# Two first pieces in whole float32, and weights split over four stages instead of three

## The chip, the cores and the metric

The kernel runs on one core of a Trainium2 chip. The metric is the device time of one execution in microseconds (us). A core has five engines that run side by side, each through its own instructions in the order in which they are written: TensorE (PE in the profile; its weight loads are PEld), VectorE (DVE), ScalarE (ACT), GpSimd (POOL) and SyncE (SP, which issues every transfer here). They wait for each other through semaphores.

## The reference

```python
scores = q @ k.transpose(0, 1, 3, 2) / 8             # 4 batches, 8 heads, 576 tokens, 64 a head
kth = np.partition(scores, -32, axis=-1)[..., -32:-31]
attn = softmax(np.where(scores >= kth, scores, -1e9))  # the 32 largest of each row
x = (attn @ v) as 2304 tokens of 512
x = (sigmoid(x @ w_gate) * (x @ w_val)) @ w_out       # 512 -> 1536 -> 512
out = np.maximum(x @ w_in, 0) ** 2 @ w_out2           # 512 -> 2048 -> 512
```

All of it is float32.

## The kernel before

The 2304 tokens are worked in six **pieces** of 192, 384, 448, 512, 512 and 256 tokens. The attention of a piece runs ahead of its two feed-forward layers, and the attention of later pieces runs beside the layers of earlier ones.

**Attention** goes by 144 *tiles* of 128 query rows, for one head, or for two heads with 64 rows each. A tile's scores are made on PE (`score`, L402), copied out by ACT (L529), and seven passes on DVE find its 32 largest (`select`, L661 and L663). ACT and POOL turn that into masked and normalised probabilities (L534 to L551, L728, L733). PE transposes them (`turn`, L418) and multiplies them by v (`times_v`, L438). ACT copies the result to x (`copy_x`). The program is written in 150 *slots*. In slot s, DVE selects tile s, PE makes the scores of tile s + 3, and POOL masks tile s - 2 and normalises tile s - 3.

**The layers** go by 68 *blocks* of weights (512 x 128) for each piece: 24 `gate` and `val`, 12 `y`, 16 `h`, 16 `out`. PE takes a block in two halves. `MLP_AT` names the slot in which a piece's layers begin (16, 41, 69, 101, 133 and 149), and `shares` deals its halves out evenly over the slots up to the next piece's. Those of the last piece come after everything (`REST`). Three PSUM banks take the sums in turn, and DVE, ACT and POOL empty them (`evac`).

The first piece multiplies whole float32 values (L483). The others split each operand into two float32r parts, high and low, and sum three products (L497 to L499). Weights get to that form once: ACT writes the high part of a block (L575), POOL the low part (L723), and SP stores both to `w_split` in HBM (`store_parts`, L337); later pieces load them from there (L332). A third of the blocks is split before the first piece's layers, a third during that piece, right after PE has used the block whole, and a third during the second piece, five blocks ahead of use.

Blocks pass through a **ring** of eight places. SP walks the blocks in order. At block k it first loads block k + 7 into the place that block k - 1 leaves, and then stores the parts of block k if it is one of the split ones:

```python
load_weights(k - 1 + RING)
...
if c == 0 and k in SPLIT_OF:
    store_parts(k)
```

`load_weights` waits in `wait_place` until PE is done with the block that held the place (`blk_done`) and, where that block was split, until its store has landed (`w_stored`, L301). `store_parts` waits for POOL's low part.

Of the kernel before, what the change touches and what calls it, by code (L numbers as in the profile page):

```python
# [25 lines left out]
CHUNK_BLOCKS = (3, 6, 7, 8, 8, 4)  # L26
NC = len(CHUNK_BLOCKS)
WIDTH = [B64 * n for n in CHUNK_BLOCKS]
# [66 lines left out]
JOBS = [(None, n, True, True) for n in range(0, NB, 3)]  # L95
NPRE = len(JOBS)
JOBS += [(c, n, c < 2 and c == n % 3 - 1, c == 0 or c == 1 and n % 3 == 2) for c in range(NC) for n in range(NB)]

SPLITS = sorted((k for k in range(len(JOBS)) if JOBS[k][2]), key=lambda k: k - (AHEAD + 0.5 if JOBS[k][0] == 1 else 0))
# [11 lines left out]
MLP_AT = [CHUNK_END[c] + (6 if c else 5) for c in range(NC)]  # L111
# [60 lines left out]
for _c in range(1, NC):  # L172
# [10 lines left out]
def attention_mlps(nc, qk, v, w, w_split, out):  # L183
    with ExitStack() as ctx:
# [15 lines left out]
        probs_h = sb("probs_h", [P, SEQ + B64])  # L200
# [11 lines left out]
        g_hi = sb("g_hi", [P, NJ2, NMAX], F32R)  # L212
        g_lo = sb("g_lo", [P, NJ2, NMAX], F32R)
# [11 lines left out]
        T0, LAST, PV, ACC0 = 2, 4, P, 5  # L225

# [14 lines left out]
        def probs_of(t):  # L241
            u, part = TILES[t]
            return probs_h[:, 0:SEQ] if part == 2 else probs[:, RANK[u] % 2, part, :]
# [62 lines left out]
        def _(sp):  # L306
# [33 lines left out]
            def mlp_dma(blocks):  # L340
                for c, n in blocks:
                    kind, m, i, parts = BLOCKS[n]
                    k = NPRE + c * NB + n

                    load_weights(k - 1 + RING)
                    if k + AHEAD in SPLIT_OF and JOBS[k + AHEAD][0] == 1:
# [34 lines left out]
        def _(pe):  # L381
# [24 lines left out]
            def turn(u):  # L406
                pe.wait_ge(norm_done, END[u] + 1)
                wait(pe, pt_copied, u)

                wait(pe, s_copied, max([t + 1 for t in range(NT) if TILES[t][1] == 1  # L410
                                        and FIRST_OF[TILES[t][0]] - SCORE <= END[u] + TURN], default=0))

                wait(pe, x_done, u)
                half = UNITS[u][4]
                both = probs_h if half else probs[:, RANK[u] % 2, :, :].rearrange("p h c -> p (h c)")
# [26 lines left out]
            def mlp_half(c, half):  # L442
                n = half // 2
                kind, t, i, parts = BLOCKS[n]
                if i == 0 and half % 2 == 0:
                    a = c * NA + ACC_OF[n] - NACC
                    before, (kind_a, ta) = a // NA, ACCS[a % NA]
                    if a < 0:
                        pass
                    elif kind_a == "gate":  # L450
                        pe.wait_ge(tanh_done, before * NJ1 + ta + 1)
                    elif kind_a == "val":
                        pe.wait_ge(gv_done, before * NJ1 + ta + 1)
                    elif kind_a == "y":
                        if before == 0:
                            pe.wait_ge(y_hi_done, ta + 1)
                        else:
                            pe.wait_ge(y_lo_done, (before - 1) * NM + ta + 1)
                    elif kind_a == "h":
                        pe.wait_ge(relu_done, before * NJ2 + ta + 1)  # L460
                    else:
                        pe.wait_ge(out_copied, before * NM + ta + 1)
                job = NPRE + c * NB + n
                if half % 2 == 0:
                    if c == 1 and job in SPLIT_OF:
                        pe.wait_ge(w_lo_done, SPLIT_OF[job] + 1)
                    else:
                        pe.wait_ge(ring_loaded[job % RING], 16 * (job // RING + 1))
                dst = acc(c, n)
                for kt in range(half % 2 * KT // 2, (half % 2 + 1) * KT // 2):  # L470
                    k = i * KT + kt
                    first, final = k == 0, k == parts * KT - 1
                    if c == 0:
                        if n == 0:
                            pe.wait_ge(x_done, X_UNIT[0][k] + 1)
                        elif kind == "y" and t == 0:
                            pe.wait_ge(gv_done, k + 1)
                        elif kind == "h" and t == 0:
                            pe.wait_ge(y_hi_done, k + 1)
                        elif kind == "out" and t == 0:  # L480
                            pe.wait_ge(sq_done, k + 1)
                        data = g0 if kind in ("y", "out") else y0 if kind == "h" else x0
                        mm = nc.tensor.matmul(dst, whole(job)[:, kt * P:kt * P + P], data[:, k, 0:WIDTH[c]],  # L483
                                              start=first, stop=final)
                        continue
                    if n == 0:
                        pe.wait_ge(x_lo_done, (c - 1) * NM + k + 1)
                    elif kind == "y" and t == 0:
                        pe.wait_ge(gv_lo_done, (c - 1) * NJ1 + k + 1)
                    elif kind == "h" and t == 0:  # L490
                        pe.wait_ge(y_lo_done, (c - 1) * NM + k + 1)
                    elif kind == "out" and t == 0:
                        pe.wait_ge(sq_lo_done, (c - 1) * NJ2 + k + 1)
# [30 lines left out]
        def _(act):  # L524
# [39 lines left out]
            def copy_x(u):  # L564
                c, g, p, i, half, col = UNITS[u]
                act.wait_ge(pv_done, u + 1)
                if c > 1:

                    act.wait_ge(x_lo_done, (c - 2) * NM + p + 1)
                x, n = (x0 if c == 0 else xf), (B64 if half else P)  # L570
# [11 lines left out]
            def evac(c, n):  # L582
# [3 lines left out]
                if k + AHEAD in SPLIT_OF and JOBS[k + AHEAD][0] == 1:  # L586
                    split_weights(k + AHEAD)
                if c == 0 and k in SPLIT_OF:
                    split_weights(k)
                if i == parts - 1 and kind != "val":  # L590
# [8 lines left out]
                    elif kind == "y":  # L599
                        y = y0 if c == 0 else xy_hi  # L600
# [8 lines left out]
                if c > 0 and 2 <= n <= 2 * NJ1 and n % 2 == 0:  # L609
# [3 lines left out]
                if c > 0 and H0 < n <= OUT0:  # L613
# [36 lines left out]
        def _(dve):  # L650
# [27 lines left out]
            def evac(c, n):  # L678
                kind, t, i, parts = BLOCKS[n]
                n_w = WIDTH[c]  # L680
                if kind == "val":
                    dve.wait_ge(blk_done, c * NB + n + 1)
                    dve.wait_ge(tanh_done, c * NJ1 + t + 1)
                    if c > 0 and t >= 2:
                        dve.wait_ge(gv_lo_done, (c - 1) * NJ1 + t - 1)
                    gv = g0[:, t, 0:n_w] if c == 0 else full_buf[:, t % 2, 0:n_w]
# [3 lines left out]
                if c > 0 and kind == "y" and i == parts - 1:  # L690
# [4 lines left out]
                if c > 0 and H0 + 2 <= n < OUT0 + 2:  # L695
                    j = n - H0 - 2
                    dve.wait_ge(sq_hi_done, (c - 1) * NJ2 + j + 1)
# [20 lines left out]
        def _(pool):  # L718
            def split_weights(k):
                pool.wait_ge(w_hi_done, SPLIT_OF[k] + 1)  # L720
                if JOBS[k][0] == 0:
# [15 lines left out]
            def split_x(c, p):  # L737
                pool.wait_ge(x_hi_done, (c - 1) * NM + p + 1)
# [4 lines left out]
            def evac(c, n):  # L743
                n_w = WIDTH[c]
                k = NPRE + c * NB + n
                if k + AHEAD in SPLIT_OF and JOBS[k + AHEAD][0] == 1:
                    split_weights(k + AHEAD)
                if c == 0 and k in SPLIT_OF:
                    split_weights(k)
                if c > 0 and 2 <= n <= 2 * NJ1 and n % 2 == 0:  # L750
                    j = n // 2 - 1
                    pool.wait_ge(gv_hi_done, (c - 1) * NJ1 + j + 1)
# [3 lines left out]
                if H0 <= n < OUT0:  # L756
                    j = n - H0
                    pool.wait_ge(relu_done, c * NJ2 + j + 1)
                    if c > 0 and j >= 2:
                        pool.wait_ge(sq_lo_done, (c - 1) * NJ2 + j - 1)  # L760
                    elif c > 0:
                        pool.wait_ge(gv_lo_done, (c - 1) * NJ1 + NJ1 - 1 + j)
                    sq = g0[:, j, 0:n_w] if c == 0 else full_buf[:, j % 2, 0:n_w]
# [4 lines left out]
            nc.gpsimd.memset(probs_h[:, :], 0.0).then_inc(const_step, 1)  # L768
# [69 lines left out]
```

## Time and profile before

| | |
|---|---|
| runs of the kernel | 1252.79, 1248.31, 1250.70 us; median 1250.7 |
| the profiled execution | 1252.19 us, of which 1250.4 us from the first instruction to the last |
| busy in that span | PE 1169.2, DVE 848.4, ACT 740.7, POOL 626.3 us |
| mean granted TensorE clock | 0.978 of full speed |
| moved by DMA | 270 MB |

Busy time overlaps between engines; a busy PE also counts the drain of one matmul beside the start of the next. A stage of the program is best read by its own window: how long it lasted, which engine was busy in all of it, and what the others waited for.

### The profile page before, as it was taken

The page shows a single profiled execution, that of the slowest core. Times are in us where ns is not written, and L with a number is a line of the kernel's source. Part 1 is how long each engine was busy: PE and PEld are TensorE (multiplying, and loading weights), DVE is VectorE, ACT ScalarE, POOL GpSimd, SP SyncE. Part 2 cuts the span into 40 slices and gives each one's busy share as a digit, 9 for nine tenths or more (in the row PEclk, how much of TensorE's full clock was granted, in tenths as well). Part 3 has the DMA queues.
Part 4 walks back from the last instruction along what each step waited for, and adds up shares of the span by engine and source line. Part 5 has one row for each costly group of instructions (what it writes and reads, how often), then busy time and mean ns, then how long its engine had stood idle before and what let it go on. Part 6 is the DMA issues. An engine that isn't in the chain of part 4 may idle for free.

```text
span 1250.4 us, 21797 instructions
## 1 busy us (share of the span) xinstructions
PE 1169.2 (94%) x7520; PEld 991.9 (79%) x7520; DVE 848.4 (68%) x1756; ACT 740.7 (59%) x1758; POOL 626.3 (50%) x539
## 2 busy tenths in 40 slices
PE   3469989869999999999999999999999999999999
PEld 2248877769999898888888777777778788888999
DVE  7988988737779977788997667688864445610121
ACT  5777778557768756666776666467654443531221
POOL 4875668646648845553664445356543333530220
PEclk9769999989999999999999999999999999999999
DMA  7874667686665785655456555454555545556997
GB/s 262 313 266 143 230 209 225 204 298 225 224 228 199 246 309 192 198 199 170 160 191 230 200 168 191 168 185 153 175 193 194 178 160 181 176 189 212 365 369 263
DMA packets 89245, 270.13 MB, mean 216 GB/s; under 512 B 9904, under 2 KB 15024, under 8 KB 89136
## 3 DMA queue, kind: packets, MB, share of 16 engines
q1 hardware_dynamic: 89136, 268.74, 62.7%
q8 instruction: 61, 1.00, 0.4%
q14 instruction: 48, 0.39, 0.1%
HBM read 228.33 MB, written 40.37 MB: 215 GB/s over the span
## 4 chain that ended last, share of the span: by engine, by line
PE 80%; ACT 6%; POOL 4%; DMA 4%; DVE 4%; issue 2%; SPq 1%; ACTq 0%; DVEq 0%; POOLq 0%
PE ps L497 21%; PE ps L499 19%; PE ps L498 19%; PE ps L438 6%; PE ps L402 5%; PE ps L418 5%; PE ps L483 3%; DMA w_split<-ring 2%; POOL below L728 2%; DVE work L663 2%; DVE top L661 1%; POOL ring L723 1%; ACT scores L529 1%; DMA ring<-w_in 1%; ACT probs L548 1%
## 5 line engine op out<-in xcount | busy, mean ns | idle before, releaser
L728 POOL TENSOR_TENSOR below<-scores,below 128x576 f32<-128x576 f32 x144 | 205.2, 1425 | 297.9 <-ACT below L541 285.5
L661 DVE MAX8 top<-work 128x8 f32<-128x576 f32 x432 | 312.9, 752 | 5.0
L497 PE MATMUL ps<-xy_hi,ring 128*128 128x512 f32 (+3 forms) x800 | 292.1, 365 | 0.3 <-ACT act_buf L597 0.3
L499 PE MATMUL ps<-xy_hi,ring 128*128 128x512 f32 (+3 forms) x800 | 283.2, 354 | 0.0
L498 PE MATMUL ps<-xy_lo,ring 128*128 128x512 f32 (+3 forms) x800 | 283.2, 354 | 0.0
L663 DVE MATCH_REPLACE8 work<-top,work 128x576 f32<-128x576 f32 x288 | 213.8, 742 | 0.0
L497 PE MATMUL ps<-g_hi,ring 128*128 128x512 f32 (+3 forms) x560 | 203.0, 363 | 0.0
L499 PE MATMUL ps<-g_hi,ring 128*128 128x512 f32 (+3 forms) x560 | 197.8, 353 | 0.0
L498 PE MATMUL ps<-g_lo,ring 128*128 128x512 f32 (+3 forms) x560 | 197.6, 353 | 0.0
L497 PEld LDWEIGHTS ps<-xy_hi,ring 128*128 128x128 f32 x800 | 151.4, 189 | 24.8 <-issue 9.7
L687 DVE SCALAR_TENSOR_TENSOR full_buf<-act_buf,ps 128x512 f32<-128x512 f32 (+3 forms) x60 | 35.5, 591 | 193.1 <-PE ps L499 176.7
L499 PEld LDWEIGHTS ps<-xy_hi,ring 128*128 128x128 f32 x800 | 151.4, 189 | 15.9
L498 PEld LDWEIGHTS ps<-xy_lo,ring 128*128 128x128 f32 x800 | 151.7, 190 | 14.1
L733 POOL TENSOR_TENSOR probs<-probs,rinv 128x576 f32<-128x576 f32 x128 | 153.2, 1197 | 16.3 <-DVE rinv L676 15.9
L548 ACT ACTIVATE probs<-below,nbias 128x576 f32<-128x576 f32 x128 | 100.1, 782 | 66.6 <-POOL below L728 65.0
L753 POOL TENSOR_TENSOR g_lo<-full_buf,g_hi 128x512 fp32r<-128x512 f32 (+3 forms) x60 | 65.8, 1096 | 126.3 <-ACT g_hi L612 126.3
L402 PE MATMUL ps<-heads_in 64*128 64x288 f32 (+1 forms) x640 | 103.3, 469 | 17.6 <-ACT scores L529 8.0
L497 PEld LDWEIGHTS ps<-g_hi,ring 128*128 128x128 f32 x560 | 105.6, 189 | 16.9 <-issue 7.0
L418 PE MATMUL ps<-ident,probs 128*128 128x128 f32 x576 | 79.9, 288 | 40.5 <-POOL probs L733 20.9
L499 PEld LDWEIGHTS ps<-g_hi,ring 128*128 128x128 f32 x560 | 105.6, 189 | 11.0
L723 POOL TENSOR_TENSOR ring<-ring 128x512 fp32r<-128x512 f32 x68 | 87.2, 1289 | 53.9 <-ACT ring L575 43.2
L534 ACT ACTIVATE below<-scores,top 128x576 f32<-128x576 f32 x144 | 111.7, 776 | 3.8 <-DVE top L661 3.5
(56 smaller groups left out, 1749.9 us busy)
## 6 DMA issues: line engine op xcount, KB each, us to landing
ring<-w_split SPq DMA_DIRECT2D x318, 512.0 KB, 3.7
w_split<-ring SPq DMA_DIRECT2D x68, 512.0 KB, 4.2
ring<-w_in SPq DMA_DIRECT2D x113, 256.0 KB, 3.4
vt<-v_in SPq DMA_DIRECT2D x16, 480.0 KB, 5.3
heads_in<-qk_in SPq DMA_DIRECT2D x16, 336.0 KB, 4.8
vt<-v_in SPq DMA_DIRECT2D x16, 320.0 KB, 4.1
heads_in<-qk_in SPq DMA_DIRECT2D x16, 240.0 KB, 3.8
heads_in<-qk_in SPq DMA_DIRECT2D x8, 368.0 KB, 5.6
```

The source lines that it names most:

```text
L402: mm = nc.tensor.matmul(ps[out_rows, score_bank(t) + half, 0:HALF], heads_in[rows, r, P * i:P * i + n], heads_in[rows, r, q:q + HALF], sta ...
L418: mm = nc.tensor.transpose(dst, both[:, P * k:P * k + P], ident[:, :])
L497: nc.tensor.matmul(dst, w_hi, hi[:, k, 0:WIDTH[c]], start=first, stop=False)
L498: nc.tensor.matmul(dst, w_hi, lo[:, k, 0:WIDTH[c]], start=False, stop=False)
L499: mm = nc.tensor.matmul(dst, w_lo, hi[:, k, 0:WIDTH[c]], start=False, stop=final)
L534: nc.scalar.activation(below[:, t % 2, :], scores[:, t % PLACES, :], ACT.Sign, bias=top[:, t % 4, TOPK - 1:TOPK], scale=-1.0).then_inc(sig ...
L548: nc.scalar.activation(probs_of(t), below[:, t % 2, :], ACT.Exp, bias=nbias[:, t % 4:t % 4 + 1], scale=SCALE, accum_out=rsum[:, t % 4:t % ...
L661: nc.vector.max(out=best, in_=sc if step == 0 else wk).then_inc(sel_step[t % 2], 1)
L663: nc.vector.match_replace(out=wk, in_to_replace=best, in_values=sc if step == 1 else wk, imm_value=-3.0e38).then_inc(sel_step[t % 2], 1)
L723: nc.gpsimd.tensor_tensor(out=place(k)[:, 1, :], in0=whole(k), in1=place(k)[:, 0, :].bitcast(F32), op=ALU.subtract).then_inc(w_lo_done, 1)
L728: nc.gpsimd.tensor_tensor(out=below[:, t % 2, :], in0=scores[:, t % PLACES, :], in1=below[:, t % 2, :], op=ALU.subtract).then_inc(mask_don ...
L733: nc.gpsimd.tensor_tensor(out=probs_of(t), in0=probs_of(t), in1=rinv[:, t % 4:t % 4 + 1].to_broadcast([P, SEQ]), op=ALU.mult).then_inc(nor ...
```

## The change

The pieces become 128, 192, 448, 512, 512 and 512 tokens, and the layers begin in slots 12, 24, 53, 85, 117 and 149. The first two pieces (`NW = 2`) multiply whole float32 values. The second of them keeps its x in a buffer of its own, `x1`, laid over `g_lo`, which is first written in the third piece. The weights are split in fourths: before the layers (17 blocks), during the first, the second and the third piece (17 each). `probs_h` gets two buffers. The work of one tile and of one block is as it was.

```diff
-CHUNK_BLOCKS = (3, 6, 7, 8, 8, 4)
+CHUNK_BLOCKS = (2, 3, 7, 8, 8, 8)
+NW = 2
...
-JOBS = [(None, n, True, True) for n in range(0, NB, 3)]
+CLASSES = NW + 2
+JOBS = [(None, n, True, True) for n in range(0, NB, CLASSES)]
...
-JOBS += [(c, n, c < 2 and c == n % 3 - 1, c == 0 or c == 1 and n % 3 == 2) for c in range(NC) for n in range(NB)]
+JOBS += [(c, n, c + 1 == n % CLASSES, c < NW or c == NW and n % CLASSES == CLASSES - 1)
+         for c in range(NC) for n in range(NB)]
...
-MLP_AT = [CHUNK_END[c] + (6 if c else 5) for c in range(NC)]
+MLP_AT = [CHUNK_END[c] + (5 if c < NW else 6) for c in range(NC)]
...
-        each = 2 * (WIDTH[c] / 0.6 + 6) if c == 0 else 6 * max(WIDTH[c] / 2.33 + 10, 110)
+        each = 2 * (WIDTH[c] / 0.6 + 6) if c < NW else 6 * max(WIDTH[c] / 2.33 + 10, 110)
...
-        probs_h = sb("probs_h", [P, SEQ + B64])
+        probs_h = sb("probs_h", [P, 2, SEQ + B64])
...
+        with nc.sbuf_tensor("x1", [P, NM, NMAX], F32) as x1:
+            pass
...
+        def x_of(c):
+            return (x0, x1)[c] if c < NW else xf
...
-                    if c == 0 and k in SPLIT_OF:
+                    if c < NW and k in SPLIT_OF:
                         store_parts(k)
...
-                    if c == 0:
+                    if c < NW:
                         if n == 0:
-                            pe.wait_ge(x_done, X_UNIT[0][k] + 1)
+                            pe.wait_ge(x_done, X_UNIT[c][k] + 1)
```

Elsewhere `c == 0` becomes `c < NW`, `c == 1` becomes `c == NW`, and counts of semaphores that start with the first split piece start at `NW`.

On PE, the start of the first piece's layers. Before, from the transposes of tile 9 on; the L483 rows are the layers, counted as the program writes them (the trace has two records for each float32 multiplication), with x as the moving operand:

```order
L418 MATMUL ps<-ident,probs 128x128 x9
L438 MATMUL ps<-pt,vt 64x128 x10
L418 MATMUL ps<-ident,probs_h 128x128 x5
L402 MATMUL ps<-heads_in 128x288 x4
L438 MATMUL ps<-pt,vt 64x64 x10
L483 MATMUL ps<-x,ring 128x192 x14
L418 MATMUL ps<-ident,probs 128x128 x9
L483 MATMUL ps<-x,ring 128x192 x2
L402 MATMUL ps<-heads_in 128x288 x4
L438 MATMUL ps<-pt,vt 64x128 x10
L483 MATMUL ps<-x,ring 128x192 x20
```

The same place after the change, where L428, L448, L412 and L493 are the lines that were L418, L438, L402 and L483:

```order
L428 MATMUL ps<-ident,probs 128x128 x9
L412 MATMUL ps<-heads_in 128x288 x4
L448 MATMUL ps<-pt,vt 64x128 x10
L493 MATMUL ps<-x,ring 128x128 x26
L428 MATMUL ps<-ident,probs 128x128 x9
L493 MATMUL ps<-x,ring 128x128 x6
L412 MATMUL ps<-heads_in 64x288 x4
L448 MATMUL ps<-pt,vt 64x128 x10
L493 MATMUL ps<-x,ring 128x128 x14
L428 MATMUL ps<-ident,probs_h 128x128 x5
L493 MATMUL ps<-x,ring 128x128 x8
```

The layers now begin after four units of probabilities instead of eight, on 128 columns instead of 192, and each stretch between two pieces of attention work holds more of them.

On SP, the middle of the first piece's layers. Before, `ring<-w_in` being the load of a whole block, `w_split<-ring` the store of a split one:

```order
L328 DMA ring<-w_in 128x512 x3
L337 DMA w_split<-ring 128x1024
L328 DMA ring<-w_in 128x512 x3
L337 DMA w_split<-ring 128x1024
L328 DMA ring<-w_in 128x512 x3
L337 DMA w_split<-ring 128x1024
L328 DMA ring<-w_in 128x512
L312 DMA heads_in<-qk_in 128x736 x2
L328 DMA ring<-w_in 128x512 x2
L337 DMA w_split<-ring 128x1024
```

After, with L338 and L347 for L328 and L337:

```order
L338 DMA ring<-w_in 128x512 x4
L347 DMA w_split<-ring 128x1024
L338 DMA ring<-w_in 128x512 x4
L347 DMA w_split<-ring 128x1024
L338 DMA ring<-w_in 128x512 x2
L322 DMA heads_in<-qk_in 128x544 x2
L338 DMA ring<-w_in 128x512 x2
L347 DMA w_split<-ring 128x1024
```

Between two stores there are now four loads instead of three, and the same order runs through the second piece as well.

## Rows read from the trace of the kernel before

**Rows 1.** The page: busy us of each engine, share of the span, instructions.

```profile
PE 1169.2 (94%) x7520; PEld 991.9 (79%) x7520; DVE 848.4 (68%) x1756; ACT 740.7 (59%) x1758; POOL 626.3 (50%) x539
```

**Rows 2.** Windows by stage: length, busy by engine, clock, DMA share, GB/s.

```profile
0.00:95.50 95.50, 46.45 (x313) 30.26 (x313) 82.23 (x176) 66.64 (x154) 63.90 (x57) 0.79 0.78 275
95.50:257.70 162.20, 141.92 (x1007) 123.24 (x1006) 132.61 (x290) 116.64 (x293) 103.71 (x94) 0.97 0.63 209
257.70:463.60 205.90, 199.19 (x1387) 181.03 (x1385) 164.66 (x342) 143.44 (x345) 132.39 (x112) 0.99 0.70 243
463.60:690.80 227.20, 225.73 (x1418) 194.57 (x1417) 186.70 (x387) 151.41 (x356) 117.24 (x97) 1.00 0.58 194
690.80:920.00 229.20, 228.07 (x1393) 177.50 (x1393) 171.54 (x351) 146.24 (x338) 113.30 (x89) 1.00 0.53 179
920.00:1149.60 229.60, 229.60 (x1203) 187.41 (x1198) 93.97 (x180) 93.17 (x209) 77.13 (x64) 1.00 0.55 182
1149.60:1250.40 100.80, 98.23 (x817) 97.92 (x816) 16.68 (x32) 23.20 (x65) 18.64 (x28) 1.00 0.89 328
```

**Rows 3.** Waits of SP's queue from 143.8 to 249.2: total us, times, longest.

```profile
SPq L301 <- DMA w_split<-ring: 67.7, 14, 6.2
```

**Rows 4.** Timeline of SP's queue in the first piece: start, length, issue.

```profile
113.16 0.33 SPq L337 DMA_DIRECT2D w_split<-ring  x1
115.81 1.28 SPq L328 DMA_DIRECT2D ring<-w_in  x3
...
143.77 1.28 SPq L328 DMA_DIRECT2D ring<-w_in  x3
...
164.00 1.28 SPq L328 DMA_DIRECT2D ring<-w_in  x3
165.32 0.43 SPq L337 DMA_DIRECT2D w_split<-ring  x1
170.28 0.33 SPq L328 DMA_DIRECT2D ring<-w_in  x1
...
249.22 0.32 SPq L332 DMA_DIRECT2D ring<-w_split  x1
```

**Rows 5.** The chain that ended last, 95 to 280: two of its links.

```profile
157.63 2.73 DMA ring<-w_in
...
214.64 6.61 DMA w_split<-ring
```

**Rows 6.** DVE timeline: first pass on tiles 12 and 16; below, that pass from 102.9 to 181.

```profile
68.65 0.74 DVE L661 MAX8 top<-scores 128x8 f32<-128x576 f32 x1
...
93.30 0.74 DVE L661 MAX8 top<-scores 128x8 f32<-128x576 f32 x1
...
L661 DVE MAX8 top<-scores x15: 740/743/744, 103.0 to 180.9; 128x8 f32<-128x576 f32 x15
```

**Rows 7.** PE timeline: the first layer matmuls, and 36 in a row without a wait.

```profile
95.47 4.23 PE L483 MATMUL ps<-x,ring 128*128 128x192 f32 x24
...
118.09 6.12 PE L483 MATMUL ps<-x,ring 128*128 128x192 f32 x36
124.05 1.15 PE L418 MATMUL ps<-ident,probs 128*128 128x128 f32 x9
```

**Rows 8.** PE timeline: first and last of 20 neighbours of 512 columns.

```profile
1130.14 0.39 PE L498 MATMUL ps<-g_lo,ring 128*128 128x512 f32 x1
...
1134.46 0.39 PE L499 MATMUL ps<-g_hi,ring 128*128 128x512 f32 x1
```

**Rows 9.** Windows: within the last piece, and around the second piece's first matmul.

```profile
1180.00:1220.00 40.00, 40.00 (x335) 39.94 (x334) 9.08 (x17) 11.30 (x32) 9.41 (x15) 1.00 0.98 368
...
250.00:275.00 25.00, 16.43 (x97) 14.66 (x97) 8.60 (x20) 10.99 (x26) 9.84 (x8) 0.86 0.86 305
```

**Rows 10.** Timeline of the end: PE's last matmul, and the last output's transfer.

```profile
1247.55 0.28 PE L499 MATMUL ps<-g_hi,ring 128*128 128x256 f32 x1
...
1248.28 0.34 SPq L352 DMA_DIRECT2D out<-act_buf  x1
```

More of the change, by code:

```diff
@@ L94 @@
 AHEAD = 5
-JOBS = [(None, n, True, True) for n in range(0, NB, 3)]
+CLASSES = NW + 2
+JOBS = [(None, n, True, True) for n in range(0, NB, CLASSES)]
 NPRE = len(JOBS)
-JOBS += [(c, n, c < 2 and c == n % 3 - 1, c == 0 or c == 1 and n % 3 == 2) for c in range(NC) for n in range(NB)]
-SPLITS = sorted((k for k in range(len(JOBS)) if JOBS[k][2]), key=lambda k: k - (AHEAD + 0.5 if JOBS[k][0] == 1 else 0))
+JOBS += [(c, n, c + 1 == n % CLASSES, c < NW or c == NW and n % CLASSES == CLASSES - 1)
+         for c in range(NC) for n in range(NB)]
+SPLITS = sorted((k for k in range(len(JOBS)) if JOBS[k][2]), key=lambda k: k - (AHEAD + 0.5 if JOBS[k][0] == NW else 0))
 SPLIT_OF = {k: r for r, k in enumerate(SPLITS)}
@@ L171 @@
     HEADS_AT.setdefault(max(FIRST_TILE[_g - 1] - 3, 0), []).append(_g)
-for _c in range(1, NC):
+for _c in range(NW, NC):
     for _p in range(PAIRS):
@@ L242, in probs_of @@
             u, part = TILES[t]
-            return probs_h[:, 0:SEQ] if part == 2 else probs[:, RANK[u] % 2, part, :]
+            return probs_h[:, RANK[u] % 2, 0:SEQ] if part == 2 else probs[:, RANK[u] % 2, part, :]
         def place(k):
@@ L414, in turn @@
                 half = UNITS[u][4]
-                both = probs_h if half else probs[:, RANK[u] % 2, :, :].rearrange("p h c -> p (h c)")
+                both = probs_h[:, RANK[u] % 2, :] if half else probs[:, RANK[u] % 2, :, :].rearrange("p h c -> p (h c)")
                 for k in range(KFULL + 1 if half else NBLK):
@@ L454, in mlp_half @@
                     elif kind_a == "y":
-                        if before == 0:
-                            pe.wait_ge(y_hi_done, ta + 1)
+                        if before < NW:
+                            pe.wait_ge(y_hi_done, before * NM + ta + 1)
                         else:
-                            pe.wait_ge(y_lo_done, (before - 1) * NM + ta + 1)
+                            pe.wait_ge(y_lo_done, (before - NW) * NM + ta + 1)
                     elif kind_a == "h":
@@ L464, in mlp_half @@
                 if half % 2 == 0:
-                    if c == 1 and job in SPLIT_OF:
+                    if c == NW and job in SPLIT_OF:
                         pe.wait_ge(w_lo_done, SPLIT_OF[job] + 1)
@@ L566, in copy_x @@
                 act.wait_ge(pv_done, u + 1)
-                if c > 1:
-                    act.wait_ge(x_lo_done, (c - 2) * NM + p + 1)
-                x, n = (x0 if c == 0 else xf), (B64 if half else P)
+                if c > NW:
+                    act.wait_ge(x_lo_done, (c - NW - 1) * NM + p + 1)
+                x, n = x_of(c), (B64 if half else P)
                 nc.scalar.activation(x[:, p, col:col + n], ps[:, LAST, PV:PV + n], ACT.Copy).then_inc(x_done, 1)
@@ L585, in evac @@
                 k = NPRE + c * NB + n
-                if k + AHEAD in SPLIT_OF and JOBS[k + AHEAD][0] == 1:
+                if k + AHEAD in SPLIT_OF and JOBS[k + AHEAD][0] == NW:
                     split_weights(k + AHEAD)
-                if c == 0 and k in SPLIT_OF:
+                if c < NW and k in SPLIT_OF:
                     split_weights(k)
@@ L599, in evac @@
                     elif kind == "y":
-                        y = y0 if c == 0 else xy_hi
+                        y = y0 if c < NW else xy_hi
                         nc.scalar.activation(y[:, t, 0:n_w], acc(c, n), ACT.Copy, scale=0.5).then_inc(y_hi_done, 1)
@@ L608, in evac @@
                         nc.scalar.activation(act_buf[:, t % 2, 0:n_w], acc(c, n), ACT.Copy).then_inc(out_copied, 1)
-                if c > 0 and 2 <= n <= 2 * NJ1 and n % 2 == 0:
+                if c >= NW and 2 <= n <= 2 * NJ1 and n % 2 == 0:
                     j = n // 2 - 1
@@ L612, in evac @@
                     nc.scalar.activation(g_hi[:, j, 0:n_w], full_buf[:, j % 2, 0:n_w], ACT.Copy).then_inc(gv_hi_done, 1)
-                if c > 0 and H0 < n <= OUT0:
+                if c >= NW and H0 < n <= OUT0:
                     j = n - H0 - 1
@@ L683, in evac @@
                     dve.wait_ge(tanh_done, c * NJ1 + t + 1)
-                    if c > 0 and t >= 2:
-                        dve.wait_ge(gv_lo_done, (c - 1) * NJ1 + t - 1)
-                    gv = g0[:, t, 0:n_w] if c == 0 else full_buf[:, t % 2, 0:n_w]
+                    if c >= NW and t >= 2:
+                        dve.wait_ge(gv_lo_done, (c - NW) * NJ1 + t - 1)
+                    gv = g0[:, t, 0:n_w] if c < NW else full_buf[:, t % 2, 0:n_w]
                     nc.vector.scalar_tensor_tensor(out=gv, in0=act_buf[:, t % 2, 0:n_w],
@@ L689, in evac @@
                                                    op1=ALU.mult).then_inc(gv_done, 1)
-                if c > 0 and kind == "y" and i == parts - 1:
+                if c >= NW and kind == "y" and i == parts - 1:
                     dve.wait_ge(y_hi_done, c * NM + t + 1)
@@ L720, in split_weights @@
                 pool.wait_ge(w_hi_done, SPLIT_OF[k] + 1)
-                if JOBS[k][0] == 0:
+                if JOBS[k][0] is not None and JOBS[k][0] < NW:
                     pool.wait_ge(blk_done, k - NPRE + 1)
@@ L758, in evac @@
                     pool.wait_ge(relu_done, c * NJ2 + j + 1)
[L759 to L763, printed above, removed]
+                    if c >= NW and j >= 2:
+                        pool.wait_ge(sq_lo_done, (c - NW) * NJ2 + j - 1)
+                    elif c >= NW:
+                        pool.wait_ge(gv_lo_done, (c - NW) * NJ1 + NJ1 - 1 + j)
+                    sq = g0[:, j, 0:n_w] if c < NW else full_buf[:, j % 2, 0:n_w]
                     nc.gpsimd.tensor_tensor(out=sq, in0=act_buf[:, j % 2, 0:n_w],
@@ L767, in _ @@
             nc.gpsimd.memset(ident[:, :], 0.0)
-            nc.gpsimd.memset(probs_h[:, :], 0.0).then_inc(const_step, 1)
+            nc.gpsimd.memset(probs_h[:, :, :], 0.0).then_inc(const_step, 1)
             pool.wait_ge(const_step, 1)
```

32 lines of the change are left out of this document (16 added, 16 removed).

## The prediction

> **What bounds the kernel now.** The page comes first: PE is busy 94% of the span [rows 1]. That is an average over unlike stages, so the next view is the windows by stage [rows 2]. From 463.6 us on PE is busy in 225.7 of 227.2 us, then 228.1 of 229.2, 229.6 of 229.6, 98.2 of 100.8: there PE's amount of work is the time. Before that it is not. Up to 95.5 us there is only attention, with PE busy 46.5 us. In the first piece's layers PE is busy 141.9 of 162.2 us, in the second piece's 199.2 of 205.9.
>
> Who sets the pace of the first piece? SP's waits say it [rows 3]: from 143.8 to 249.2 us SP stood 67.7 us, 14 times, until a store to `w_split` had landed. The timeline shows the cycle [rows 4]: three loads at 164.00, a store at 165.32, and the next load only at 170.28, because its place in the ring is the one being stored; SP issues in order, so every load behind it stands too. From 143.77 to 249.22 that is 15 cycles, 7.03 us each for three blocks, 2.34 us a block, attention's own loads included. PE needs less. 36 neighbouring records take 5.96 us [rows 7], 0.1655 each, so a block of eight is 1.32 us. Attention costs PE 1.83 us a slot: a pass of 512 columns takes 4.32 / 19 = 0.2274 us [rows 8], a piece has 816, and the two pieces from 690.8 to 1149.6 us with 48 slots give (458.8 - 371.1) / 48. At the stage's mean of 162.2 / 25 = 6.5 us a slot, 16 slots passed in those 105 us, so PE had 45 x 1.32 + 16 x 1.83 = 89 us to do. The chain agrees: it runs through a store at 214.64 and a load at 157.63 [rows 5].
>
> **The change, stage by stage.** All sums are against the span of 1250.4 us.
>
> *Start of the layers.* It moves from slot 16 to slot 12. DVE starts tile 12 at 68.65 and tile 16 at 93.30 [rows 6], and the first layer matmul follows the latter by 2.2 us [rows 7]. I put the new start at 70 us: 25.5 gained. Six blocks fewer are split before it, which may bring 67; more and shorter head loads may cost up to 78.
>
> *First piece, 128 tokens.* Proportional to columns a record takes 0.110 us, 544 of them 60 us; if it got no shorter than at 192 columns, 90. With 12 slots of attention PE's need is 82 us (112 at most). But the piece still walks 68 blocks, with 17 stores among them, and between two stores stand four loads. The shortest cycle is 7.03 plus one issue of 0.43, that is 7.46. The longest grows with the bytes, from 1.31 to 1.57 MB: 8.4. I take the 0.26 MB at the 368 GB/s that the last piece reaches [rows 9], 0.71 us: 7.75 us for four blocks, against PE's 4 x 82 / 68 = 4.8. SP therefore sets this stage. The last block's load stands behind the fifteenth store: 4.5 us to the first store, 14 cycles, and 11 us for that store, three issues, the landing and the last block. That is 4.5 + 108.5 + 11 = 124 us (120 to 134). Behind the late blocks on PE stand the scores of the next tiles, so DVE idles here: 12 slots in 124 us.
>
> The Trainium skill ("DMA: Bandwidth & Descriptors", Anatomy of one DMA) fits a DMA, on the GpSimd path, as about 2.0 us plus bytes over 436 GB/s, which is an estimate of 3.2 us for this store. The store at 113.16 landed within 2.65 us, near that, but with three loads just ahead of it in the queue it takes 5.0. By the skill's price the stage would last some 90 us and the sum would be 1232.
>
> *Second piece, 192 tokens in float32.* PE: 544 x 0.1655 = 90, plus 29 slots x 1.83 = 53: 143 us. The stores' chain, 17 cycles of 7.75, is 132 us and hidden. The pace is DVE's: from 103.0 to 180.9 us, beside a piece of the same width, 14 slots took 77.9 us, 5.56 each [rows 6]; 29 slots are 161.5 us. Bounds: 29 slots of seven passes of 0.743 us are 151, and the first piece's 6.5 us a slot would make 188.
>
> *Third piece, 448 tokens, 32 slots.* The same piece took 227.2 us before [rows 2]. It now also has the 17 splits ahead of use that the second piece had, and that piece began badly: from 250 to 275 us PE was busy 16.4 us [rows 9], because the ring was empty behind the stores. Here the ring is full before it, as the second piece leaves the chain slack. I add 7: 234 (228 to 244).
>
> *Fourth and fifth piece, 512 each.* PE-bound before and after; they now carry 64 slots of attention instead of 48: 371.1 + 64 x 1.83 = 488 us. DVE's 64 x 5.56 us are hidden.
>
> *Last piece, 512 instead of 256.* No attention is left: 816 x 0.2274 = 185.5 us. The tail after PE's last matmul, 2.9 us [rows 10], grows to about 3.5 with twice the output: 189, against 100.8. DMA, at 0.98 share before [rows 9], gets slack, but PE was never short of a block there, so that pays nothing.
>
> `x1`, the second `probs_h` and the shifted counts add no instruction. POOL clears twice as much of `probs_h` at the start, behind the first transfer of heads; uncovered that would shift the start by its own length, within the start's bounds.
>
> Sum: 70 + 124 + 161.5 + 234 + 488 + 189 = 1266.5 us, 16 more than the span before. Or in two halves: the start gains 25.5, the float32 pieces take 285.5 where one took 162.2, and what is left takes 911 instead of 992.7: -25.5 + 123.3 - 81.7 = +16. The profiled execution lay 1.8 us over its span and 1.5 over the median of the runs, so the median should be about 1267.
>
> **The rivals.**
>
> *The stores land as if alone (faster).* If each lands within 3 us, as at 113.16, a cycle is 5 x 0.43 + 3.0 = 5.2 us, the chain needs 4.5 + 14 x 5.2 + 9 = 86 us, near PE's 82, and the stage lasts about 90. It decides from a cycle of 4.8 us down that PE alone sets the stage. Everything else unchanged: 1232. For it: the trace has such stores. Against it: they came when SP had waited for something else first; in saturation the 14 waits averaged 4.8 us. 0.18. The Trainium skill's fit, above, amounts to this case.
>
> *The second piece falls behind.* At the first piece's mean of 6.5 us a slot it takes 188 us: 1293. For it: waits in order on five engines add up. Against it: the later slots of that stage were held by SP's chain, which here has 30 us of slack. 0.12.
>
> *The clock falls.* With PE idle for a third of the first piece, it may be granted the lower of its levels, 1.2 GHz, in much of it. From 250 to 275 us, with PE busy 16.4 us, the mean was 0.86; before the layers it was 0.79 [rows 2]. At half clock throughout, PE needs 2 x 82 = 164 us, 40 more than SP: 1306. Short drops are covered by SP's waits. 0.06.
>
> *The forecast*, stores in saturation: 0.64, in a range of its own from 1249 to 1284 (the bounds above, not all at one end at once).
>
> **The numbers.** A change under 0.3%, 3.8 us, cannot be told from none here, as the three runs lie 0.36% apart. Faster, under 1247: the first rival and a sliver of the forecast, 0.20. Within: the forecast's lower edge, and a first piece halfway to the rival, 0.12. Slower: the rest, 0.68. The range from 1238 to 1290 leaves out most of the first rival, the third, and the upper end of the second.
>
> **What would show it.** The first layer matmul at 67 to 78 us. SP's waits for `w_split` stores filling most of the first piece, cycles near 7.75 us with four loads, PE waiting for `ring<-w_in` there and DVE busy about half. The second piece's layers begin near 194 us and last about 160, with DVE near full. PE busy all through from the third piece on, the last piece 189 us. The prediction is wrong if cycles in the first piece come near 5 us, or if the second piece is paced by anything but DVE.

## The result, and the profile after

The change makes the kernel slower: 1291.5 us median of four runs (1289.06 to 1293.95) against 1250.3, a ratio of 1.0334 (95% interval 1.0313 to 1.0355). The direction was forecast, the size was not: 41 us instead of 16, and 1.5 us beyond the range. The profiled execution took 1291.94 us, with a span of 1290.1.

The page, with the rows that answer to [rows 1] and the slices of PE's busy time:

```profile
PE 1185.0 (92%) x7248; PEld 975.1 (76%) x7248; DVE 838.9 (65%) x1736; ACT 734.1 (57%) x1726; POOL 618.2 (48%) x523
...
PE   2587667999989999999999999999999999999999
```

The windows by stage, in the columns of [rows 2]: before the layers, the first, second and third piece, the fourth and fifth together, the last piece with the tail.

```profile
0.00:77.60 77.60, 35.79 (x188) 23.33 (x188) 63.24 (x133) 48.32 (x108) 47.00 (x43) 0.81 0.75 267
77.60:208.90 131.30, 97.67 (x819) 87.51 (x817) 64.87 (x146) 65.66 (x170) 58.16 (x58) 0.93 0.66 216
208.90:375.40 166.50, 149.45 (x1132) 128.53 (x1130) 148.23 (x329) 123.78 (x315) 104.46 (x94) 0.98 0.66 219
375.40:613.10 237.70, 229.83 (x1419) 197.54 (x1417) 188.61 (x387) 162.63 (x379) 142.37 (x117) 0.99 0.62 218
613.10:1101.90 488.80, 487.18 (x2886) 385.13 (x2885) 345.56 (x711) 296.85 (x689) 234.09 (x186) 1.00 0.52 171
1101.90:1290.10 188.20, 185.11 (x817) 153.01 (x815) 28.43 (x32) 36.90 (x65) 32.06 (x28) 1.00 0.54 178
```

Beside the forecast's terms of 70, 124, 161.5, 234, 488 and 189 us stand 77.6, 131.3, 166.5, 237.7, 488.8 and 188.2. The two PE-bound terms fit within 1 us. The first four are all too small, by 7.6, 7.3, 5.0 and 3.7 us, together 23.6.

In the first piece SP's waits, as in [rows 3], are for the stores again: 76.7 us in 15 waits.

```profile
SPq L311 <- DMA w_split<-ring: 76.7, 15, 6.7
SPq L347 <- POOL ring L733: 7.2, 2, 5.5
```

PE's own waits in that stage show what this does, which before had been 7.7 us between 143.8 and 249.2:

```profile
PE ps L493 <- DMA ring<-w_in: 30.5, 21, 3.4
```

SP's timeline, to be read as [rows 4], has the cycle of four loads and a store. The first store of the piece is at 85.15, 7.5 us after the first matmul; the fifteenth, at 196.09, comes 14 cycles later, (196.09 - 85.15) / 14 = 7.92 us each:

```profile
85.15 0.33 SPq L347 DMA_DIRECT2D w_split<-ring  x1
...
161.52 1.75 SPq L338 DMA_DIRECT2D ring<-w_in  x4
163.31 0.43 SPq L347 DMA_DIRECT2D w_split<-ring  x1
169.13 1.75 SPq L338 DMA_DIRECT2D ring<-w_in  x4
...
196.09 0.44 SPq L347 DMA_DIRECT2D w_split<-ring  x1
```

PE's timeline at the start shows the third group's scores waiting for their heads. At the start of the second piece it shows a wait for a block, and behind it a longer one for ACT; at the start of the third a wait for ACT alone:

```profile
14.90 2.29 PE L412 MATMUL ps<-heads_in 64*128 64x288 f32 x8 [5.67 <-DMA heads_in<-qk_in]
...
77.61 2.65 PE L493 MATMUL ps<-x,ring 128*128 128x128 f32 x17
...
208.90 1.47 PE L493 MATMUL ps<-x,ring 128*128 128x192 f32 x8
212.54 1.70 PE L493 MATMUL ps<-x,ring 128*128 128x192 f32 x9 [2.17 <-DMA ring<-w_in]
...
222.61 1.33 PE L412 MATMUL ps<-heads_in 64*128 64x288 f32 x4 [4.91 <-ACT pt L572]
...
381.74 0.76 PE L412 MATMUL ps<-heads_in 64*128 64x288 f32 x4 [4.23 <-ACT pt L572]
```

Both waits for ACT lead back to SP's queue. In the second piece ACT could not empty one of its first sums into `act_buf`, because an output of the first piece was still to be read from there, and SP issued that transfer only after it had stood for a store. In the third piece ACT stood for a block that it was to split. SP's timeline, then ACT's:

```profile
212.13 0.43 SPq L347 DMA_DIRECT2D w_split<-ring  x1
217.37 0.80 SPq L338 DMA_DIRECT2D ring<-w_in  x2
218.22 0.43 SPq L362 DMA_DIRECT2D out<-act_buf  x1
```

```profile
220.99 0.33 ACT L607 ACTIVATE act_buf<-ps 128x192 f32<-128x192 f32 x1 [5.17 <-DMA out<-act_buf]
...
377.70 1.15 ACT L585 ACTIVATE ring<-ring 128x512 fp32r<-128x512 f32 x2 [3.32 <-DMA ring<-w_in]
```

### The profile page after: what moved, and what is told of

Read it like the earlier page. It is cut to its first block, busy times and chain, and to the rows that moved or that the text cites. A ratio compares the mean times of both kernels' runs of the same rounds, so it can differ in the third digit from the quotient of the medians.

```text
span 1290.1 us, 21141 instructions
## 1 busy us (share of the span) xinstructions
PE 1185.0 (92%) x7248; PEld 975.1 (76%) x7248; DVE 838.9 (65%) x1736; ACT 734.1 (57%) x1726; POOL 618.2 (48%) x523
## 4 chain that ended last, share of the span: by engine, by line
PE 77%; ACT 8%; DMA 7%; POOL 4%; issue 3%; DVE 1%; SPq 1%; ACTq 0%; POOLq 0%; DVEq 0%
PE ps L507 19%; PE ps L509 18%; PE ps L508 18%; PE ps L448 7%; PE ps L412 6%; PE ps L493 6%; PE ps L428 4%; DMA ring<-w_in 4%; DMA w_split<-ring 3%; POOL below L738 2%; ACT below L544 1%; ACT scores L539 1%; ACT probs L558 1%; ACT ring L585 1%; ACT below L551 1%
## 5 line engine op out<-in xcount | busy, mean ns | idle before, releaser
L507 PE MATMUL ps<-xy_hi,ring 128*128 128x512 f32 (+1 forms) x640 | 253.0, 395 | 0.0
L509 PE MATMUL ps<-xy_hi,ring 128*128 128x512 f32 (+1 forms) x640 | 246.1, 385 | 0.0
L508 PE MATMUL ps<-xy_lo,ring 128*128 128x512 f32 (+1 forms) x640 | 246.1, 385 | 0.0
L507 PE MATMUL ps<-g_hi,ring 128*128 128x512 f32 (+1 forms) x448 | 176.6, 394 | 0.0
L509 PE MATMUL ps<-g_hi,ring 128*128 128x512 f32 (+1 forms) x448 | 172.2, 384 | 0.0
L508 PE MATMUL ps<-g_lo,ring 128*128 128x512 f32 (+1 forms) x448 | 172.0, 384 | 0.0
L507 PEld LDWEIGHTS ps<-xy_hi,ring 128*128 128x128 f32 x640 | 120.3, 188 | 28.4 <-issue 8.3
L509 PEld LDWEIGHTS ps<-xy_hi,ring 128*128 128x128 f32 x640 | 120.3, 188 | 22.1
L412 PE MATMUL ps<-heads_in 64*128 64x288 f32 (+1 forms) x640 | 104.0, 467 | 30.5 <-ACT pt L572 17.1
L697 DVE SCALAR_TENSOR_TENSOR full_buf<-act_buf,ps 128x512 f32<-128x512 f32 (+1 forms) x48 | 32.0, 668 | 149.9 <-PE ps L509 149.9
L448 PEld LDWEIGHTS ps<-pt,vt 128*64 128x64 f32 x1600 | 86.2, 145 | 35.5 <-issue 24.1
L763 POOL TENSOR_TENSOR g_lo<-full_buf,g_hi 128x512 fp32r<-128x512 f32 (+1 forms) x48 | 60.3, 1257 | 109.0 <-ACT g_hi L622 109.0
L671 DVE MAX8 top<-scores 128x8 f32<-128x576 f32 x144 | 107.0, 743 | 5.9 <-ACT scores L539 5.9
L774 POOL TENSOR_TENSOR full_buf<-act_buf 128x512 f32<-128x512 f32 (+1 forms) x64 | 66.2, 1039 | 92.1 <-ACT act_buf L615 81.5
```

What stands on the lines that cost most here:

```text
L412: mm = nc.tensor.matmul(ps[out_rows, score_bank(t) + half, 0:HALF], heads_in[rows, r, P * i:P * i + n], heads_in[rows, r, q:q + HALF], sta ...
L448: mm = nc.tensor.matmul(ps[DH * h:DH * h + DH, LAST, PV:PV + n], vt[:, g % 2, v_at:v_at + DH], pt[:, u % 2, p_at:p_at + n], start=(k == 0) ...
L507: nc.tensor.matmul(dst, w_hi, hi[:, k, 0:WIDTH[c]], start=first, stop=False)
L508: nc.tensor.matmul(dst, w_hi, lo[:, k, 0:WIDTH[c]], start=False, stop=False)
L509: mm = nc.tensor.matmul(dst, w_lo, hi[:, k, 0:WIDTH[c]], start=False, stop=final)
L671: nc.vector.max(out=best, in_=sc if step == 0 else wk).then_inc(sel_step[t % 2], 1)
```

## The experiments

The theory: SP's wait for each store, in order ahead of the next loads, paces the first piece and makes the second begin late. Rivals: the engines' waits on each other pace it; the transfers' own time does; the width of the piece does. Stage lengths below run from a piece's first layer matmul to the next one's. They come from one profiled execution of each kernel; five of the kernels (no stores, thirds, both short ones and the 128 columns) were run only once. Where an edit leaves a stage alone, it repeats well: with the change the third piece took 237.7, and in three kernels edited elsewhere 237.7 to 238.4 us. The start of the layers scatters more, from 76.2 to 78.8 us in eight kernels with the same work before it.

**No stores in the first piece.**

```diff
-JOBS += [(c, n, c + 1 == n % CLASSES,
+JOBS += [(c, n, 0 < c and c + 1 == n % CLASSES,
...
+KEPT = [n - (n % CLASSES == 1) for n in range(NB)]
...
-                             w_split[n, :, :])
+                             w_split[KEPT[n], :, :])
```

> The changed kernel without any split or store during the first piece; later pieces load a neighbour's stored block in place of those 17, so their values are not the reference's while every transfer keeps its size. If SP's wait for the stores paces the first piece, that piece falls from 131 us to PE's need, 82 to 95 us, and SP waits for PE there instead; the second piece then begins on a full ring and loses its slow first slots, 166 to about 156 us. Span about 1240 to 1250. If the engines' waits on each other in order pace it, the piece stays over 115 us and the span over 1270.

The span fell to 1237.5 us, just under the expected. Windows of the first three pieces:

```profile
76.20:164.90 88.70, 85.56 (x819) 79.42 (x817) 64.73 (x146) 55.55 (x153) 36.64 (x41) 0.99 0.74 240
164.90:322.00 157.10, 146.51 (x1132) 126.10 (x1130) 148.22 (x329) 123.80 (x315) 104.81 (x94) 1.00 0.67 223
322.00:560.50 238.50, 231.06 (x1420) 198.28 (x1417) 188.61 (x387) 162.65 (x379) 142.34 (x117) 0.98 0.61 215
```

and SP's longest wait in the first of them:

```profile
SPq L339 <- PE ps L494: 51.5, 57, 3.2
```

SP now waits for PE, and the first piece takes 88.7 us with PE busy 85.6 of them. So the 17 stores (with their splits) cost the first piece 131.3 - 88.7 = 42.6 us and the second 166.5 - 157.1 = 9.4 more, though the second piece's own stores are unchanged. The third piece, behind those, keeps its 238.

**Thirds again, widths unchanged.**

```diff
-CLASSES = NW + 2
+CLASSES = NW + 1
...
-    SPLIT_AT.setdefault(2 + _k // 2, []).append(_k)
+    SPLIT_AT.setdefault(2 + 10 * _k // NPRE, []).append(_k)
```

> The changed kernel with the weights split in thirds again (before the layers, in the first and in the second piece, up to three a slot before the layers), widths unchanged. The first two pieces then have 23 stores each with three loads between them. If the number of stores paces the first piece, whatever its width, it rises from 131 us to 150 to 160, near the 162 that a piece of 192 tokens took before; the second piece is then near its own limit by the stores, 165 to 175. If the width paces it, it stays near 131 us. The third piece should lose its 4 us over the old one.

Span 1309.7 us. The first two windows:

```profile
79.10:231.10 152.00, 108.25 (x819) 96.42 (x818) 65.16 (x146) 68.18 (x176) 65.49 (x64) 0.85 0.69 224
231.10:401.10 170.00, 150.18 (x1130) 128.61 (x1129) 148.68 (x329) 127.24 (x322) 111.32 (x100) 0.98 0.67 230
```

The first two came as expected, the third piece, at 231.6 us, lost 6.1. A piece of 128 tokens with 23 stores takes 152 us, nearer to the 162 of 192 tokens with 23 stores [rows 2] than to its own 131 with 17: the number of stores weighs more than the width, 21 us against 10. Splitting in fourths was by itself a gain, of 20 us.

**The reload four blocks later, behind the next store.** In this edit and the next of its kind, `split_late(k)` is true for the blocks that are split after use.

```diff
+                    if not split_late(k - 1):
-                    load_weights(k - 1 + RING)
+                        load_weights(k - 1 + RING)
...
                         store_parts(k)
+                    if split_late(k - CLASSES):
+                        load_weights(k - CLASSES + RING)
```

> The changed kernel with the same work and the same stores; only SP's order differs: the load into the place of a block that is being stored is issued after the next store, four blocks later, so that the three loads behind it no longer stand. If the in-order wait is the cause, the first piece takes 90 to 105 us, the second about 156, and the span is 1245 to 1262. If the transfers themselves are the limit (their bytes and landing times), the first piece stays near 125 to 131 us and the span within 10 us of 1290.

1294.4 us, 1.035 times the kernel before (1.030 to 1.039): no gain, the first piece 132.2 us and the second 175.4. That looks like the rival, transfers as the limit. But SP's waits in the piece had changed their object:

```profile
SPq L347 <- POOL ring L739: 76.1, 17, 8.3
SPq L338 <- PE ps L499: 11.7, 21, 1.3
```

SP no longer waits for a store, it waits for POOL's low part of the next block to be stored. That block's load now lay behind a store in the queue, only four blocks ahead, so PE got it late (PE waited for loads 30.7 us in that piece), POOL after PE, and the store after POOL: another loop through the same place, of the same length.

**The reload three blocks later, ahead of the next store.**

```diff
+                    if not split_late(k - 1):
-                    load_weights(k - 1 + RING)
+                        load_weights(k - 1 + RING)
+                    if split_late(k - 3):
+                        load_weights(k - 3 + RING)
...
                         store_parts(k)
```

> The changed kernel, same work; the load into the place of a stored block is issued three blocks later, ahead of the next store and not behind it as in the run before. If the stand-still of SP in order was the cost, and the last try only swapped it for a load that lay behind a store and reached PE late, a cycle of four blocks shrinks from 7.9 to about 6 us, the first piece to 98 to 112 us and the span to 1250 to 1270. If the transfers' own time paces the cycle, the piece stays over 125 us.

The profiled span was 1250.5 us. Its pieces:

```profile
77.10:184.00 106.90, 91.55 (x821) 83.70 (x818) 65.61 (x147) 64.84 (x170) 57.45 (x57) 0.95 0.81 271
184.00:342.00 158.00, 146.71 (x1132) 126.02 (x1130) 148.21 (x329) 124.63 (x318) 105.17 (x94) 1.00 0.69 230
342.00:573.40 231.40, 226.49 (x1420) 195.09 (x1417) 187.66 (x387) 161.96 (x378) 142.47 (x117) 1.00 0.63 222
```

With every store and every byte kept, 24.4 us go from the first piece, 8.5 from the second and 6.3 from the third. The cycle of four blocks is 6.3 us. The transfers were not the limit; DMA now moves 271 GB/s there instead of 216. Not all of the cost is gone: the piece is 18 us longer than without stores, and SP still waited 32.0 us for stores in it and 20.5 us for POOL. The profiled execution was the fastest of five (1252.3 to 1263.1); their median, 1258.8, is 1.0077 times the kernel before (1.0042 to 1.0112).

**The first piece's splits moved to the third piece.**

```diff
-JOBS += [(c, n, c + 1 == n % CLASSES, c < NW or c == NW and n % CLASSES == CLASSES - 1)
+JOBS += [(c, n, c == 1 and n % 4 == 2 or c == NW and n % 2 == 1, c < NW or c == NW and n % 2 == 1)
```

> The changed kernel with the first piece's 17 splits moved into the third piece (34 there, five blocks ahead of use); nothing is left out. First piece 87 to 95 us, second about 157, third 242 to 252 as each 17 splits cost it about 6 us; the span 1240 to 1252, so the change without stores in its first piece is even with the kernel before or up to 0.8% faster. If splits ahead of use cost as much as those in the first piece, the third piece grows by 40 us and nothing is won.

1245.4 us, 0.9962 of the kernel before (0.9945 to 0.9979). First piece 90.3, second 157.1, third 241.0: with 17 more splits ahead of use that piece is 2.5 us longer than in the run without stores, not 6. Pieces and widths of the change, with the stores out of the first piece, are thus a small gain over the kernel before, and 46 us better than as written.

**Heads ahead of half of the first weights.**

```diff
-            for k in range(RING):
+            for k in range(RING // 2):
                 load_weights(k)
...
+                if s == 1:
+                    for k in range(RING // 2, RING):
+                        load_weights(k)
```

> The changed kernel with four of the first eight weight loads issued one slot later, behind the heads of the third and fourth group, for which PE waits 5.7 us now. If that wait is what made the slots before the layers 5.6 to 7 us long instead of 5.1, the first layer matmul comes at 70 to 73 us instead of 77.6 and the span falls by 4 to 7 us. If ACT and POOL are simply full in these slots, the start stays at 76 to 78 us and the span too.

1289.4 us, 1.0318 (1.0272 to 1.0364) of the kernel before; the span was 1285.2 instead of 1290.1, but the medians are only 2.1 us apart, within the scatter of either kernel. The layers began at 73.9 us instead of 77.6, just above the expected: by this run the wait for heads explains 3.7 of the 7.6 us by which the start missed.

**Moved splits and heads together.** The edits of the last two runs in one kernel.

> The changed kernel with the first piece's splits in the third piece and with four of the first weight loads behind the heads, nothing left out. The two gains lie in different stages: start 73 to 74 us, first piece 89 to 91, the rest as with the splits moved alone; span 1236 to 1241, 0.6 to 1.1% under the kernel before. If the earlier start is eaten by the first piece, the span stays at 1242.

1242.2 us, 0.9938 (0.9919 to 0.9957). The start is at 74.8 where the moved splits alone had 77.1, so here the heads are worth 2.3 us; the first piece takes 90.3 us. The two gains add up, nearly.

**Selection of the second piece's tiles cut short.**

```diff
-                sc, wk, tp = scores[:, t % PLACES, :], work[:, t % 2, :], top[:, t % 4, :]
+                cols = B64 if step > 3 and MLP_AT[1] <= t < MLP_AT[2] else SEQ
+                sc, wk, tp = scores[:, t % PLACES, :], work[:, t % 2, 0:cols], top[:, t % 4, :]
```

> The changed kernel with the last three selection passes cut to 64 columns for the 29 tiles of the second piece's slots (its masks are not the reference's). If DVE paces the second piece, its 166.5 us fall by 20 or more, to PE's or the stores' need, 140 to 147 us, and the span to about 1268. If the stores or PE pace it, it stays over 160 us. The first piece keeps its 131 us either way, as DVE idles there.

The second piece stayed at 166.3 us, with DVE idle a third of it:

```profile
210.00:376.30 166.30, 150.41 (x1130) 129.68 (x1130) 105.08 (x329) 123.41 (x315) 103.68 (x94) 0.97 0.67 220
```

DVE, which the prediction named, does not pace this piece alone. It now waited, 31 us between 230 and 375, for the row sums of ACT.

**POOL's mask cut short as well.**

```diff
-                                     scale=KILL).then_inc(below_done, 1)
+                                     scale=0.0 if MLP_AT[1] <= t < MLP_AT[2] else KILL).then_inc(below_done, 1)
...
+                cols = B64 if MLP_AT[1] <= t < MLP_AT[2] else SEQ
-                nc.gpsimd.tensor_tensor(out=below[:, t % 2, :], in0=scores[:, t % PLACES, :], in1=below[:, t % 2, :],
+                nc.gpsimd.tensor_tensor(out=below[:, t % 2, 0:cols], in0=scores[:, t % PLACES, 0:cols], in1=below[:, t % 2, 0:cols],
```

> As the run with short selection, and POOL's mask of the second piece's tiles cut to 64 columns as well (with no masking there, so those values are not the reference's). If with DVE relieved the loop from ACT through POOL's mask back to ACT paced the second piece, about 1.2 us a slot goes: 166 falls to 152 to 158 us, where PE's own need of 143 and the slow first slots stand. If PE or the stores paced it, it stays at 163 us or more.

```profile
208.90:367.80 158.90, 148.24 (x1132) 129.40 (x1130) 107.17 (x335) 123.10 (x315) 74.52 (x94) 0.98 0.68 221
```

7.6 us less, just above the expected 152 to 158 us. The third piece gave 5.7 back (243.4; why was not tried), so the span was 1288.2.

**The second piece's layers on 128 of its columns.**

```diff
+DONE = [P if c == 1 else WIDTH[c] for c in range(NC)]
...
-                        mm = nc.tensor.matmul(dst, whole(job)[:, kt * P:kt * P + P], data[:, k, 0:WIDTH[c]],
+                        mm = nc.tensor.matmul(dst, whole(job)[:, kt * P:kt * P + P], data[:, k, 0:DONE[c]],
```

> The changed kernel with the layers of the second piece on 128 of its 192 columns (the other 64 are not computed), attention, blocks and stores unchanged. PE needs 28 us less there. If PE paces the second piece, it falls from 166 us to 150 or less. If attention's engines (DVE with ACT and POOL) pace it, it stays at 158 to 167 us: PE's relief is worth nothing.

```profile
209.50:372.70 163.20, 127.14 (x1130) 108.15 (x1129) 147.16 (x329) 121.49 (x315) 102.02 (x94) 0.96 0.66 223
```

With PE relieved of 22 us of busy time (and DVE, ACT and POOL of 1 to 2.4 us, as they empty narrower sums) the piece is 3.3 us shorter. So no one engine paces it: DVE relieved alone gives 0.2 us, PE alone 3.3, DVE and POOL's mask together 7.6. That fits attention as the pace, with DVE (busy 131.4 of the 135 us from 235 to 370) and the loop through ACT and POOL about equally long, and PE a few us behind. It is not shown how long the loop is by itself, as POOL's mask was not cut with DVE's work kept.

**The kernel before, with its stores out of the way.** Two kernels: its first piece's splits moved to the second piece,

```diff
-JOBS += [(c, n, c < 2 and c == n % 3 - 1, c == 0 or c == 1 and n % 3 == 2) for c in range(NC) for n in range(NB)]
+JOBS += [(c, n, c == 1 and n % 3 > 0, c == 0 or c == 1 and n % 3 > 0) for c in range(NC) for n in range(NB)]
```

> The kernel before with the first piece's splits moved into its second piece (45 there, five blocks ahead of use); nothing is left out. If the stores paced its first piece too, that falls from 162 to 138 to 146 us, the pace of DVE's slots (25 of 5.56) and PE's need, and the second piece's bad start goes: span 1218 to 1235. If only the changed kernel was held by its stores, the first piece stays over 155 us and the span near 1250.

and the reload of a stored place two blocks later, ahead of the next store:

```diff
+                    if not split_late(k - 1):
-                    load_weights(k - 1 + RING)
+                        load_weights(k - 1 + RING)
+                    if split_late(k - 2):
+                        load_weights(k - 2 + RING)
```

> The kernel before, same work and same stores; only the load into the place of a stored block is issued two blocks later, ahead of the next store. If SP's stand-still paced its first piece as well, that falls from 162 us to 142 to 152 and the span to 1230 to 1242. If its 162 us were attention's pace, span and piece stay within 4 us.

They took 1233.9 us, 0.9868 (0.9837 to 0.9899), and 1233.6 us, 0.9875 (0.9842 to 0.9908). First pieces of the two:

```profile
96.00:240.30 144.30, 138.55 (x1008) 121.82 (x1006) 131.88 (x290) 105.76 (x270) 77.02 (x72) 1.00 0.54 162
```

```profile
94.40:244.60 150.20, 140.31 (x1010) 122.05 (x1006) 132.30 (x292) 115.68 (x291) 103.11 (x93) 0.99 0.67 228
```

SP's stand-still had cost the kernel before some 17 us as well. With the same kind of edit in both, its pieces beat those of the change: 1233.9 against 1245.4 with the splits moved, 1233.6 against 1258.8 with later reloads. These two are the fastest of all; the change with both its float32 pieces free of stores was not run. Later reloads took 4.6 us from the second piece (201.3). Moving the splits left it at 205.3 us, although its bad start was mended. The first 25 us of that piece, in the kernel before and with the splits moved:

```profile
257.70:282.70 25.00, 20.88 (x132) 18.68 (x131) 12.28 (x28) 12.87 (x33) 12.74 (x11) 0.90 0.79 284
```

```profile
240.30:265.30 25.00, 22.61 (x159) 20.64 (x159) 16.77 (x38) 17.75 (x43) 18.25 (x16) 1.00 0.81 284
```

PE has 159 records there instead of 132. The piece as a whole is as long as before, so that lead was lost again later, beside 23 more splits.

## Why the prediction had the direction and not the size

The span missed by 23.6 us. Two terms were the right ones and too small: the start by 7.6 us and the first piece by 7.3. The other 8.7 lie in the second and third piece, and there a step failed in kind: the forecast let the stores' harm end with the piece that makes them.

- *SP's stores pace the first piece*: right, and the step on which the sign rested. The cycle of four blocks was 7.92 us, forecast 7.75; without stores the stage took 88.7 us, near the 82 that the forecast gave as PE's need. The stage missed by 7.3 us: 3 for a first store 7.5 instead of 4.5 us after the start, 2.4 for the cycles, 1.8 for the end. The 4.5 us stand on no row: the kernel before had its first store at 103.01, also 7.5 us after its first layer matmul at 95.47 [rows 7].

```profile
103.01 0.33 SPq L337 DMA_DIRECT2D w_split<-ring  x1
```

- *The stores land as if alone*: fell. 76.7 / 15 = 5.1 us a wait. The Trainium skill's fit ("DMA: Bandwidth & Descriptors", Anatomy of one DMA), by which some 3.2 us were estimated, is no price for a store with four loads ahead of it.
- *Start of the layers at 70*: the largest miss for its size, 77.6, at the very end of its bounds. It read slots from a trace in which heads came in time. With two-tile groups the third group's heads are needed sooner and stood behind eight weight loads; that is 3.7 us of it by one pair of runs and 2.3 by the other, and the start scatters by 2.6. The rest lies in slots of 5.6 to 7 us before the layers; why they are not 5.1 was not tried.
- *The second piece leaves SP behind*: the step that failed in kind. The forecast let the stores' harm end with the first piece ("29 slots are 161.5 us", "Here the ring is full before it"). The second piece lost 9.4 us, by the run without the first piece's stores. The third lost 6.3 behind the second's stores, by the run with later reloads, which kept the third's own splits. An empty ring is the smaller part of it: at the second piece's start PE waited 2.2 us for a block and 4.9 for ACT, which waited for late outputs; at the third's start it waited 4.2 us for ACT, which waited for a block to split. The forecast's reading of the kernel before ("because the ring was empty behind the stores") misses the same link: PE's 7.5 us before 255.9 were a wait for ACT, which stood 6.7 us for a block to split:

```profile
255.90 2.15 PE L418 MATMUL ps<-ident,probs 128*128 128x128 f32 x9 [7.51 <-ACT scores L529]
```

```profile
253.93 0.63 ACT L575 ACTIVATE ring<-ring 128x512 fp32r<-128x512 f32 x1 [6.74 <-DMA ring<-w_in]
```

- *Luck in the same two terms*: they missed by only 5.0 and 3.7 us because their own pace was better than forecast, 157.1 instead of 161.5 us and 231.4 instead of 234. Without the 15.7 us handed on, the span would by subtraction have been some 1274 us, inside the range. It is also by chance that the 1290.1 lies next to the 1293 of the rival in which the second piece falls behind: that rival wanted 188 us for the piece, which took 166.5.
- *DVE sets the second piece*: the size was nearly right (157 us when the ring was full, against 161.5), the reason holds only in part. DVE's work cut alone changed nothing, and by the prediction's own sign ("paced by anything but DVE") this step fell.
- *Fourth to last piece*: right within 1 us for each term. The window of the last piece shows PE busy 185.1 of 188.2, DMA at 0.54 share instead of 0.89, and that slack paid nothing, as forecast.
- *The clock*: a mean of 0.93 in the first piece, not the half that the rival needed.
- *The range*: every term came out inside its own bounds, but the range counted on them "not all at one end at once". Three of the four misses had one cause, SP's stores, and so one sign.

## What to carry to other kernels

A queue that waits in order for a store before it goes on loading pays for each store (4.8 us a wait before the change, 5.1 after), however little work stands between two; making that work smaller turns the price into the pace of the stage. Look at the queue's own waits, and when one is moved, look at what it waits for next: the first reordering only changed the wait's object. A stage that ends with its queue late hands its loss on, by missing blocks, by late outputs and by an engine that waits in order for either, so its price has to be looked for in the next stage too.

## What was not expected of the hardware

Splitting weights five blocks ahead of use, on ACT, POOL and DMA, costs a piece that PE fills little (2.5 us for 17 blocks more; 4.2 us for the 17 of the run with later reloads, whose third piece took 231.4 us against 227.2 in the kernel before), while the same 17 in the first piece cost 52 us over two pieces. And in a stage in which DVE was busy 148 of 166 us, taking 43 us of work from it changed nothing: 166.5 to 166.3.
